# Attention in a fused attention and feed-forward kernel: query blocks paired (7,8), (5,6), (3,4), (1,2), heads of a job one after the other

## What is computed

```python
scores = scale * q @ k.T                     # 576 x 576 for each of 32 heads
mask = block_i >= block_j                    # blocks of 64 positions: 9 x 9
attn = softmax(where(mask, scores, -1e9))    # sum + 1e-9
x = attn @ v                                 # to (2304, 512)
h = x @ w_in;  x = (h * sigmoid(h)) @ w_out
h = x @ w2_in; y = (h * sigmoid(1.702 * h)) @ w2_out
```

## Time and profile before

| | |
|---|---|
| median of 3 runs | 951.75 us (951.27 to 951.77) |
| profiled execution, its own time | 951.22 us |
| its span, first to last instruction | 949.4 us |
| PE busy | 931.8 us, 98% |
| mean granted TensorE clock | 0.995 |

### The profile page before, as it was taken

One profiled execution on the slowest core, in us unless ns is written; L12 is line 12 of the kernel. 1 busy time (PEld: TensorE's weight loads), 2 busy tenths in 40 slices (PEclk: granted clock), 3 DMA queues, 4 the chain that ended last, 5 costly groups with the idle time before them and its releaser, 6 DMA issues.

```text
span 949.4 us, 14419 instructions
## 1 busy us (share of the span) xinstructions
PE 931.8 (98%) x5304; PEld 796.8 (84%) x5304; DVE 534.5 (56%) x1096; ACT 385.4 (41%) x854; POOL 302.3 (32%) x408
## 2 busy tenths in 40 slices
PE   5999999999999999999999999999999999999998
PEld 4788877787778777877788888999999999999997
DVE  6788665665666556755434425454655454644443
ACT  4667534443445344544323323232443233523232
POOL 5899447664553364435717200000000000000000
PEclk8999999999999999999999999999999999999999
DMA  8554695796688863887527986434354434363431
GB/s 244 166 161 144 189 290 173 238 322 220 185 279 263 266 194 114 267 284 254 203 94 284 366 312 219 122 112 123 112 177 122 125 108 133 101 199 104 131 101 67
DMA packets 65190, 179.57 MB, mean 189 GB/s; under 512 B 7136, under 2 KB 8800, under 8 KB 59232
## 3 DMA queue, kind: packets, MB, share of 16 engines
q1 hardware_dynamic: 64688, 177.99, 59.7%
q10 hardware_dynamic: 432, 0.66, 0.2%
HBM read 130.02 MB, written 44.56 MB: 184 GB/s over the span
## 4 chain that ended last, share of the span: by engine, by line
PE 91%; DVE 3%; ACT 1%; POOL 1%; issue 0%; ACTq 0%; POOLq 0%
PE ps_y L958 20%; PE ps_y L1016 13%; PE ps_h L941 7%; PE ps_a L1017 7%; PE ps_h L943 6%; PE ps_h L942 6%; PE ps_a L921 5%; PE ps_a L909 4%; PE ps_a L989 3%; PE ps_a L992 3%; PE ps_a L991 3%; PE ps_h L989 3%; PE ps_h L992 3%; PE ps_h L991 3%; PE ps_a L889 2%; PE ps_a L861 2%
## 5 line engine op out<-in xcount | busy, mean ns | idle before, releaser
L958 PE MATMUL ps_y<-g_hi,w_hl 128*128 128x512 f32 (+1 forms) x640 | 189.5, 378 | 0.3 <-DVE g_lo L1367 0.2
L1016 PE MATMUL ps_y<-o_hi,w_out 128*128 128x512 f32 x368 | 139.9, 391 | 0.0
L958 PEld LDWEIGHTS ps_y<-g_hi,w_hl 128*128 128x128 f32 x640 | 112.2, 189 | 17.1 <-DVE g_lo L1367 0.7
L1143 ACT ACTIVATE g_f<-ps_h 128x512 f32<-128x512 f32 (+1 forms) x72 | 41.5, 576 | 192.0 <-PE ps_h L943 191.9
L958 PE MATMUL ps_y<-g_lo,w_hl 128*128 128x512 f32 (+1 forms) x320 | 118.6, 371 | 0.0
L1362 DVE SCALAR_TENSOR_TENSOR g_f<-g_f,ps_h 128x512 f32<-128x512 f32 (+1 forms) x72 | 47.3, 657 | 123.4 <-ACT g_f L1143 123.0
L941 PE MATMUL ps_h<-x_hi,w_hl 128*128 128x512 f32 (+1 forms) x288 | 113.2, 393 | 0.8 <-POOL w_hl L742 0.8
L943 PE MATMUL ps_h<-x_lo,w_hl 128*128 128x512 f32 (+1 forms) x288 | 109.2, 379 | 0.0
L942 PE MATMUL ps_h<-x_hi,w_hl 128*128 128x512 f32 (+1 forms) x288 | 108.7, 378 | 0.0
L1017 PE MATMUL ps_a<-o_hi,w_out 128*128 128x256 f32 x368 | 103.0, 280 | 0.0
L1124 ACT ACTIVATE p_sb<-ps_a,nmax 128x512 f32<-128x512 f32 (+4 forms) x128 | 72.4, 572 | 69.5 <-DVE nmax L1331 69.2
(11 more groups left out here) (138 smaller groups left out, 1906.8 us busy)
## 6 DMA issues: line engine op xcount, KB each, us to landing
w_form<-f_split SPq DMA_DIRECT2D x168, 256.0 KB, 2.7
w_hl<-w_split SPq DMA_DIRECT2D x30, 1024.0 KB, 7.4
w_raw<-w_chunks SPq DMA_DIRECT2D x42, 512.0 KB, 5.4
w_split<-w_hl SPq DMA_DIRECT2D x16, 1024.0 KB, 7.9
f_split<-stage SPq DMA_DIRECT2D x24, 512.0 KB, 5.4
o_split<-stage SPq DMA_DIRECT2D x16, 512.0 KB, 4.2
w_out<-o_split SPq DMA_DIRECT2D x16, 512.0 KB, 8.5
k_raw<-kT SPq DMA_DIRECT2D x28, 288.0 KB, 6.0
```

Of the source, the lines that this page charges most:

```text
L958: last = nc.tensor.matmul(bank_y(t, k), lhs, rhs, start=(part == 0 and f == 0 and (t > 0 or k % 2 == 0)), stop=(part == 2 and f == NF - 1) ...
L1016: nc.tensor.matmul(y_main(k), lhs, rhs[:, h, 0:512], start=begin, stop=end, skip_group_check=True)
```

## The change

- Rows of scores: a job has 8 rows, four for head 0 and then four for head 1: pair (7,8) over 576 keys (two parts of 288, each in a bank of its own), (1,2) over 192, (5,6) over 448, (3,4) over 320. All are split products. `ends`, `q_end` and `queries_end` go; `queries_high` and `queries_low` are 512 columns wide and not 384. A unit is now two rows of one head: pairs (7,8) and (1,2), or (5,6) and (3,4).
- Each row waits on `s_ex` only for the row that held its bank.
- Head 0 and head 1 are prepared apart: POOL's `keys_low`, SP's `copy_keys` and ACT's work wait for, and signal, one head each.
- Keys and values of head 1 are laid out with their blocks backwards, so that the half key tile that a pair leaves over for each head lies side by side with that of the other; one transpose takes both halves (the sixth batch, of 4 tiles, of which half the columns are copied). The number of transposes stays at 24.
- `values` has 4 whole key tiles a head (512, 384, 256, 128 queries wide) and then, for each pair and head, a 64x64 product of 64 columns with the half tile: 16 matmuls and not 10.
- Masks: 12 `affine_select` on POOL at the start and not 6, over wider tiles; two DVE memsets go.
- The places change. `START_AT` of the first four jobs is -6, 22, 50, 78 and job 4 stays at 106. For late jobs `keys_high` goes from -12, -12 to -16, -9 (head 0, head 1), `queries_high` from -9, -6 to -14, -7, `keys_low` from -7 for both to -11, -5, `copy_keys` from -9 to -13, -8.

```diff
-WIDTH = (576, 128, 512, 512, 384, 384, 256, 256)
+HEAD = (0, 0, 0, 0, 1, 1, 1, 1)
+PAIR = (3, 0, 2, 1, 3, 0, 2, 1)
+WIDTH = tuple(BLK * (2 * p + 3) for p in PAIR)
-START_AT = (-8, 19, 49, 75, 106)
+START_AT = (-6, 22, 50, 78, 106)
-UNIT_AT = ((0, 5, 11, 15), (0, 7, 13, 19))
-BATCH_AT = ((12, 13, 16, 21, 27, 29), (9, 13, 18, 20, 27, 30))
-PV_AT = (33, 32)
+UNIT_AT = ((0, 4, 8, 12), (-1, 4, 7, 15))
+SECOND_AFTER = (1, 0)
+BATCH_AT = ((8, 14, 18, 22, 26, 28), (7, 13, 19, 24, 27, 30))
+PV_AT = (30, 34)
-INVERT_AFTER = (3, 3)
-MULTIPLY_AFTER = ((4, 4), (5, 7))
-TAKE_AFTER = (1, 1)
-SPLIT_AFTER = ((1, 2), (2, 3))
+INVERT_AFTER = (2, 3)
+MULTIPLY_AFTER = ((4, 5), (3, 5))
+TAKE_AFTER = (0, 1)
+SPLIT_AFTER = ((0, 1), (2, 3))
 LOAD_AT = ((-40, -17), (-42, -24))
-PREP_AT = ((-12, -11, -7, -5, -7, -3, 0, -5, -5), (-12, -12, -9, -6, -6, -5, -4, -7, -9))
+PREP_AT = ((-21, -11, -18, -5, -12, -1, -17, -5, -10, 4), (-16, -9, -14, -7, -11, -4, -11, -5, -13, -8))
...
             def load_queries(n):
                 if n >= 2:
-                    sp.wait_ge(s_qe, before(n) + 1)
                     sp.wait_ge(s_ql, 2 * before(n) + 2)
...
-            def copy_keys(n):
-                sp.wait_ge(s_kh, 2 * (n + 1))
-                sp.dma_start(k_mask[0:D, :, :].bitcast(F32), k_both[0:D, :, :].bitcast(F32)).then_inc(s_kc, 16)
+            def copy_keys(n, h):
+                sp.wait_ge(s_kh, 2 * n + h + 1)
+                sp.dma_start(k_mask[0:D, h, :].bitcast(F32), k_both[0:D, h, :].bitcast(F32)).then_inc(s_kc[h], 16)
...
+            def scores(n, u, i):
+                h = HEAD[UNITS[u][0]]
+                if u % 2 == 0 and i == 0:
+                    pe.wait_ge(s_ql, 2 * n + h + 1)
+                    pe.wait_ge(s_kl, 2 * n + h + 1)
+                    ...
+                r = UNITS[u][i]
+                q = slice(P * PAIR[r], P * PAIR[r] + P)
+                if PAIR[r] == NPAIR - 1:
+                    parts = [(b, bank(b)[:, 0:S // 2], S // 2 * b, S // 2) for b in range(2)]
+                else:
+                    parts = [(int(PAIR[r] < 2), scored(r), 0, WIDTH[r])]
+                for b, dst, a, w in parts:
+                    a += (S - WIDTH[r]) * h
+                    taken = ROWS * n + r - 1 + (b if PAIR[r] == NPAIR - 1 else 0)
+                    if PAIR[r] and taken > 0:
+                        pe.wait_ge(s_ex, taken)
+                    nc.tensor.matmul(dst, q_twice[:, h, q], k_both[:, h, a:a + w], start=True, stop=False, ...)
+                    last = nc.tensor.matmul(dst, q_mask[:, h, q], k_mask[:, h, a:a + w], start=False, stop=True, ...)
+                last.then_inc(s_sc, 1)
...
-                for t in range(NJ):
+                for t in range(NPAIR):
                     for h in range(2):
                         d = slice(D * h, D * h + D)
-                        last = nc.tensor.matmul(bank(2)[d, OFF[t]:SQ], v_sb[:, n % 2, t, d], pt_sb[:, h, t, OFF[t]:SQ], ...)
+                        i = 2 * NPAIR - 1 - t if h else t
+                        nc.tensor.matmul(bank(2)[d, P * t:SQ], v_sb[:, n % 2, i % NPAIR, d], pt_sb[:, i, P * t:SQ], ...)
+                for p in range(NPAIR):
+                    for h in range(2):
+                        d = slice(D * h, D * h + D)
+                        q = P * p + BLK
+                        last = nc.tensor.matmul(bank(2)[d, q:q + BLK], v_half[d, n % 2, p, :], pt_half[d, p, :], ...)
```

More of the change, by code:

```diff
@@ L320, in build @@
         s_kl = sem("s_kl")
-        s_qe = sem("s_qe")
-        s_kc = sem("s_kc")
+        s_kc = [sem(f"s_kc{h}") for h in range(2)]
         s_km = sem("s_km")
@@ L634, in _ @@
                         load_keys(LOAD[1][place])
[L635 to L636 removed]
+                    for h in range(2):
+                        if place in COPY[h]:
+                            copy_keys(COPY[h][place], h)
                 if c + 5 < NF:
@@ L805, in _ @@
                 for place in range(STEP * c, STEP * (c + 1)):
-                    if place in PREP[7]:
-                        keys_low(PREP[7][place], 0)
-                        keys_low(PREP[7][place], 1)
+                    for h in range(2):
+                        if place in PREP[6 + h]:
+                            keys_low(PREP[6 + h][place], h)
                 if c + 3 < NF:
@@ L850, in early_values @@
                 last.then_inc(s_epv, 1)
[L852 to L862, removed]
-                last.then_inc(s_sc, 1)
[L864 to L892, removed]
+            def scores(n, u, i):
[3 more added lines that the diff above has]
+                    pe.wait_ge(s_kl, 2 * n + h + 1)
+                    if n < FIRST:
+                        pe.wait_ge(s_km, 2 * n + h + 1)
+                    else:
+                        pe.wait_ge(s_kc[h], 16 * (n - FIRST + 1))
+                    if n == 0 and u == 0:
+                        pe.wait_ge(s_maskd, 64)
+                r = UNITS[u][i]
+                q = slice(P * PAIR[r], P * PAIR[r] + P)
+                if PAIR[r] == NPAIR - 1:
+                    parts = [(b, bank(b)[:, 0:S // 2], S // 2 * b, S // 2) for b in range(2)]
+                else:
+                    parts = [(int(PAIR[r] < 2), scored(r), 0, WIDTH[r])]
[4 more added lines that the diff above has]
+                        pe.wait_ge(s_ex, taken)
+                    nc.tensor.matmul(dst, q_twice[:, h, q], k_both[:, h, a:a + w], start=True, stop=False,
+                                     skip_group_check=True)
+                    last = nc.tensor.matmul(dst, q_mask[:, h, q], k_mask[:, h, a:a + w], start=False, stop=True,
+                                            skip_group_check=True)
+                last.then_inc(s_sc, 1)
@@ L903, in transposes @@
                         pe.wait_ge(s_ta if by_act(n, before) else s_td, takes(n, before))
[L904 to L908, removed]
-                            last = nc.tensor.transpose(lane(n, b)[:, col:col + P], p_sb[:, a:a + P], ident[:, :])
-                            col += P
+                rows, halves = BATCHES[b]
+                tiles = [whole_tile(r, t) for r in rows for t in range(PAIR[r] + 1)]
+                tiles += [half_tile(p) for p in halves]
+                for i, tile in enumerate(tiles):
+                    last = nc.tensor.transpose(lane(n, b)[:, P * i:P * i + P], tile, ident[:, :])
                 last.then_inc(s_tr, 1)
@@ L1049, in _ @@
                     place = STEP * c + i
-                    if place in UNIT:
-                        unit(*UNIT[place])
+                    for row in range(2):
+                        if place in ROW[row]:
+                            scores(*ROW[row][place], row)
                     if place in BATCH:
@@ L1478, in _ @@
                 for h in range(2):
-                    if place in PREP[5 + h]:
-                        queries_low(PREP[5 + h][place], h)
+                    if place in PREP[4 + h]:
+                        queries_low(PREP[4 + h][place], h)
                 if i == 7 and t == NTILES - 1 and f == 1:
```

178 lines of the change are left out of this document (96 added, 82 removed).

## The result

The changed kernel takes **953.70 us** (median of 20 executions, 951.86 to 955.84) beside 951.13 of the kernel before (20 executions, 950.41 to 953.26): a ratio of 1.0022, 95% interval 1.0016 to 1.0028. It is slower by 0.2%.

What follows compares the result with a forecast made beforehand. PE, busy 98% of the span, was taken to bound the kernel. Against the profiled 951.22 us, late jobs -4.0, job 4's queries +2.3 and job 7's +1.8 gave 951.3; the forecast was 951.6, range 945.5 to 956.5.

Steps and rivals of the forecast that it cites:

- "same": Outcome case: a time between 949.85 and 953.65 us, within 0.2% of the kernel before; chance 0.38.
- PE's work in late jobs: Jobs 4 to 15: ends -1.34, values +0.11, scores +0.86, so -0.37 us a job and -4.0 in all.
- the rival of the full fp32 price: 192-column score products cost 1.8 ns a column, 0.34 us each: +9.7 us, 961 in all; chance 0.08.
- Jobs 0 to 3 "worth nothing": Savings of some 0.5 us each and start costs are hidden by a wait that POOL and a transfer fix: 0.
- Job 4's queries, the main term: Queries landing at 97.9 hold ACT ahead of g_high, delaying output of chunk 12 to 99.5: +2.3 us at place 138.
- the 3 named as the sign: Sign of being right: ACT's first queries_high of job 4 waits 3 us or more for q_raw.
- the -0.6 of less work: Places 100 to 138: ends and shape changes -1.54, values +0.11, job 4's scores +0.86, so PE does 0.6 us less.
- this pair of units: Unit 1 to unit 2 in late jobs: three PE steps of 0.7 us cover unit 1's exponentials; 0 to 0.5 a job.
- Job 7's queries: Landing near 180.8 holds ACT, so PE waits near place 194 for the copy of batch 2: +1.8 us.
- The sum: Late jobs -4.0, job 4's queries +2.3 and job 7's +1.8 against the profiled 951.22 us: 951.3.

Runs made afterwards that it cites:

- E6: E1 with queries_low of head 0 of jobs 1 to 3 four places later (-8 instead of -12): 949.14 us, kernel before 951.21.
- E1: The changed kernel with both loads of job 4's queries issued at place 73 instead of 82 and 89: 950.02 us, kernel before 951.00.
- E3: The kernel before with only job 4's two queries_high moved from places 97 and 100 to 92 and 93: 956.93 us, kernel before 951.00.
- E5: The kernel before with both loads of job 4's queries issued earlier, at place 73: 951.16 us, kernel before 951.21.
- E9: E6 with job 4's two keys_low on POOL at places 96 and 104 instead of 95 and 101: 948.82 us, kernel before 951.09.
- E7: The changed kernel with queries_low of head 0 of jobs 1 to 3 four places later, job 4's loads unmoved: 953.61 us, kernel before 951.21.
- E10: The kernel of E6 unchanged, run again beside E9 on one chip: 949.06 us, kernel before 951.09.
- E8: E6 with unit 2 of job 4 one place later (114 instead of 113): 949.83 us, ratio 0.9987 to the kernel before.
- E2: The changed kernel with job 4's preparations at the old kernel's places (queries_low one place ahead), loads unmoved: 950.84 us, kernel before 951.00.

## Why the prediction failed, step by step

Forecast was 951.6 in a range of 945.5 to 956.5, with "same" the likeliest at 0.38; measured is 953.70, in the range, and just on the slower side of the bound. What was forecast was no change, and the kernel is slower, with an interval that leaves out 1. The mechanism named as the main term was right and was mis-sized (+2.3 for +4.4); one step that was set to nothing was wrong (jobs 0 to 3, 0 for +1.4); the saving of the late jobs was 0.8 too large; and a second wait did not come (job 7, +1.8 for 0). The three misses that made the kernel slower than forecast add up to 4.3 us. That the total is off by 2.5 only, and inside the range, is luck: job 7's 1.8 covers the rest.

- **PE's work in late jobs: right.** -0.31 us a job against -0.37. Start to start, in the mean of eight jobs: `ends` -1.34 as forecast; scores +0.75, not +0.86; `values` +0.18, not +0.11; the transposes 0.00; and 0.09 that no term had, on the feed-forward matmuls around more, smaller groups. Eleven jobs give -3.4 and job 15's `values` +0.2: -3.2, where the sum had -4.0. The 192-column products and `values` of the changed kernel, answering to the earlier trace rows:

```profile
171.72 0.25 PE L920 MATMUL ps_a<-k_both,q_twice 128*128 128x192 f32 x1
171.81 0.28 PE L922 MATMUL ps_a<-k_mask,q_mask 128*128 128x192 f32 x1
171.93 0.27 PE L940 MATMUL ps_a<-ident,p_sb 128*128 128x128 f32 x1
...
194.74 2.38 PE L953 MATMUL ps_a<-pt_sb,v_sb 128*64 128x512 f32 x16
197.05 0.68 PE L960 MATMUL ps_a<-pt_half,v_half 64*64 64x64 f32 x16
197.66 0.73 PE L997 MATMUL ps_y<-g_hi,w_hl 128*128 128x512 f32 x2
```

  171.93 - 171.72 = 0.21 for two products, 0.10 each where 0.12 was taken: the rival of the full fp32 price is out. `values` takes 197.66 - 194.74 = 2.92. The Trainium skill, "TensorE: Matmul & The Clock Gate", LDWEIGHTS, gives the load of P weight columns as P/1.2 ns, by estimate 107 for 128. The mean of the two agrees; the first, 0.09 behind its predecessor, is below it, so here it is no floor for every single product.
- **Jobs 0 to 3 "worth nothing", because a wait fixed by POOL and a transfer follows: wrong in its reason, and short by 1.4 us.** The changed kernel came 1.4 us late to place 96, where 0 was forecast. POOL did not set that pace: in E6 the order of VectorE alone gives 1.15 us there against E1. The other traces say the same: the five with E6's order reach place 96 at 94.2 to 94.3 us, the four of the changed kernel without it at 95.5 to 96.5, and the three with the old attention (before, E3, E5) at 94.2 to 94.7. With VectorE in order POOL is next, at place 104 (E9). `queries_low` of head 0, 1.1 us long at its new place, delays a gate or a `g_low` in each of jobs 0 to 2. It was costed by the busy share of the engine (56%), not by what stands behind it. What was right is that a gain there is eaten by job 4's transfer: E7.
- **Job 4's queries, the main term: right in kind, +2.3 forecast, from place 96 to 136 +4.4 measured.** The wait itself: forecast 99.5, measured 100.38, as the queries landed at 98.5 and not at 97.9 (issued at 92.83, not 92.04: chunk 13's split ended 0.8 later on POOL) and `g_low` took 0.81 us and not 0.41. It is +2.3 and not +2.9 since PE was already 1.4 late at place 96. ScalarE waited 1.96 us for them, not the 3 named as the sign, since its wait of 1.21 us for the keys came first and its work had been late by PE's own delay. Not forecast: the halved clock behind the wait, 1.2 us (E1), 2.7 in E3. And the -0.6 of less work from place 100 to 136 did not come: even in E1 that stretch is 28.06 us against 27.14, +0.9. Of these 1.5 us, 0.7 is a wait at unit 2 of job 4 for the exponentials of unit 1, the longer of the two here (E1, waits from 86 to 125 us):

```profile
PE ps_a L920 <- ACT p_sb L1156: 1.3, 2, 0.7
```

  Start to start in E1 the rest lies in the transposes (+0.2), in the scores (+1.04, not +0.86), in `values` (+0.17, not +0.11) and in the feed-forward products around them (+0.15, where two changes of shape were to save 0.2); why these cost more here than in late jobs stays open. In job 4 unit 2 follows by places of the narrow tile. The prediction had looked at this pair of units for late jobs at full width, found three steps of 0.7 enough, which holds for them, and did not ask it for job 4, whose steps are half as long.
- **Job 7's queries: wrong, 0 for +1.8.** ScalarE was held as forecast, at place 188, but PE did not feel it. In E1, where PE is nearly as early as the prediction had it:

```profile
179.59 0.63 ACT L1147 ACTIVATE q_twice<-q_raw 128x512 fp32r<-128x512 f32 x1 [1.83 <-DMA q_raw<-qT]
180.13 0.62 ACT L1182 ACTIVATE g_hi<-g_f 128x512 fp32r<-128x512 f32 x1
180.65 0.58 ACT L1162 ACTIVATE pt_sb<-ps_a 128x512 f32<-128x512 f32 x1
...
181.49 0.60 PE L940 MATMUL ps_a<-ident,p_sb 128*128 128x128 f32 x4
...
DMA to landing us min/median/max: 9.2/9.7/10.2
```

  The copy of batch 2 ends at 181.23, 0.26 us before PE comes to batch 3. The step that failed is the landing: I added POOL's delay of 1.2 to the landing of before and got 180.8. The two issues were indeed 0.9 and 1.3 later (168.28 and 169.38), but the second transfer took 10.2 us and not 11.5, and the landing is the old 179.6. That it is the same is chance: E6 and E10 are one kernel, and their queries land at 178.3 and 179.2. The step is not wrong by much either. In E10 the copy ends at 180.81, and PE starts batch 3 at 180.96, 0.39 us behind the matmul before it where E9 has 0.23: some 0.16 us of the forecast wait. In the changed kernel itself PE came to batch 3 at 185.68, 4.8 later, with the copy ready at 184.96.
- **The sum.** Forecast -4.0 + 2.3 + 1.8 = +0.1 against the profiled execution; measured -3.2 + 1.4 (to place 96) + 4.4 (96 to 136) + 0 = +2.6, of 953.92 - 951.22 = 2.7. This is the account of one execution, with the halved clock; the executions without it are 1.6 us shorter (last section).

E1 to E3 show the cause of the main loss; E6 and E7 show the early one and its cover. The wait at unit 2 of job 4 is read from the trace, and E8, the one attempt on it, failed. The start's +1.4 at place 0 wasn't tried: it holds also in E6 (24.32), which is nevertheless 0.5 ahead of the kernel before at place 92, so it is covered there. (At place 8 the changed kernel is only 0.3 behind; the trace of before has half clock from 25.6 to 29.1 us.) The change with job 4's transfers in time is worth about 1 us (E1 against E5), and about 2 with VectorE's order mended too (E10 against E5); these are medians of different calls.

## What to carry to other kernels

An operation moved earlier on an in-order engine takes the engine with it when its input is a transfer: compare the landing with the new place, then look at the first thing behind it that the bottleneck wants, not at the engine's busy share. Move the load with it; here that was worth 3.7 us, more than all the work that the change saves. And a distance in places is a time only for the tile in which it was measured: check it again where steps are shorter.

## What the runs showed of the hardware that was not expected

- The granted clock fell to half in or right behind a gap of PE: after 2.1 us of wait it was 0.50 for 3.4 us (changed kernel, and 3.4 us again in E7 after 2.5 us); in E3 it fell inside a wait of 3.45 us and was low for 6.8 us. With the gap gone the traces have 1.00 there (E1, E2, E6). Behind the wait the clock then cost half to five sixths of the delay again: 1.2 on 2.4 us, 2.7 on 3.2. The length of the gap alone does not set the length of the fall: two of E3's five executions, by their mean clocks of 0.993 and 0.998, fit a fall of 3.4 us, and take 955.2 and 955.5 us where the other three, at 0.996, take 956.9 to 957.1.
- The same fall costs nothing where PE waits later anyway. E2's trace has one from 32.2 to 35.6 us, behind a wait of 1.8 us where the changed kernel has 0.65. It is 2.4 us behind the changed kernel at place 20 and 0.5 at place 44, about what it was behind at place 0 (0.4).
- The changed kernel's executions lie apart, E1's do not. A fall of 3.4 us lowers the mean clock of an execution by 0.002, and one at the start, as most traces have, by 0.005. Nine of the twenty have a mean clock of 1.0 or 0.995, as E1's have, and take 951.9 to 953.0, median 952.4; eleven have 0.993, 0.996 or 0.998 and take 953.6 to 955.8, median 953.9. So by their clocks the fall does not follow each time. Without it the change costs 1.2 us and not 2.6 (before 951.1), and E1 is 2.4 us below that group: the wait alone.
